# Banded attention: two heads share a transpose of their global columns, P*V runs three units behind, and GpSimd splits the values of pair 1

## The chip, the cores and the metric

The kernel runs on one core of a Trainium2 chip. The metric is the device time of one execution in microseconds (us), median of several. A core has five engines with queues of their own that run in program order and meet only at semaphores: TensorE (PE, with its weight loads PEld), VectorE (DVE), ScalarE (ACT), GpSimd (POOL) and SyncE (SP), which here issues transfers.

## The reference, cut to what matters

Attention with ALiBi biases over a band of 96 local keys and 8 global ones, and two feed-forward layers behind it (a dense one and a mixture of four experts), which the change does not touch.

```python
B, H, S, D = 2, 8, 768, 64
scores = scale * q @ k^T                          # per batch and head
rel = pos[:, None] - pos[None, :]
is_global = pos[None, :] < n_global               # 8
is_local = (rel >= 0) & (rel < n_local)           # 96
dist = where(is_global & ~is_local, n_local, abs(rel))
scores = where(is_global | is_local, scores - slope[h] * dist, -1e9)
a = exp(scores - max); a = a / (sum(a) + 1e-9)
x = (a @ v)                                       # then moe(x), then moe2(x)
```

## The kernel before, in words

**Tiling.** Heads go in pairs: 8 pairs, numbered m = 2i + slot. A pair is 12 units: unit u is query tile u // 2 (128 rows, six of them) of head u % 2. With the band, query tile 0 needs one block of 128 keys, tile 1 two, and tiles 2 to 5 (units 4 to 11) three: two blocks of 128 and the first GLOBAL_COLS = 32 keys. So the scores of such a unit are 288 columns wide.

**One unit's way.** PE multiplies q and k into PSUM (`scores_of_two`, L541, both heads of a tile together). DVE adds the bias and takes the row maximum (`biased`, L1109, instruction at L1117). ACT exponentiates (`expo`, L849). PE transposes blocks of 128 columns (`turn`, L578): one, two or three. The third block is the 32 global columns and 96 columns of zeros that were written once at the start (L1043). ACT copies the transposed blocks to float16 (L890), DVE writes the rest that float16 lost (L1228). PE multiplies with the values (`pv`, L597), three matmuls a block: high by high, high by low, low by high. After six units DVE divides by the sums (`output`, three steps L1149, L1153, L1157).

**Order.** It is written out by hand. In the step of unit u, PE does `turn(u)`, after odd units `scores_of_two` for u + 3 and u + 4, then `pv(u - 2)`, and in steps 0, 2, 4, 6 a transpose of the next pair's q or k (`fill`, L501). DVE does `biased(u + 2)`, the low half of unit u, and what else is due: `output` steps in u = 8, 9, 10 and in u = 1, 2, 3 of the next pair, and a piece of x (`x_low`, L1213) in u = 10 of pairs 4, 5 and 6. ACT does the copy of unit u, `expo(u + 2)`, and its own extras (`values_sum` L873, `weights_sum` L865 in units 21 to 28 and 33 to 40 of the whole count).

**The values.** Each pair's v must be scaled and split into a high and a low float16 part before its `pv`. The scale of pair 0 comes from its own maximum, the scale of all the others from the maximum over all pairs, which is known in step u = 7 of pair 0. Both maxima go over the partitions with a custom GpSimd instruction, `partition_all_reduce` (L790); DVE waits for each of them in its own queue (L1205 for the second) and makes the scale from it. Pair 0 and pair 1 are split by ACT (`values_high`, L857) and DVE (`values_low`, L1187), pairs 2 to 7 by GpSimd (L795 to L802). GpSimd's queue is: index tables by iota, `partition_all_reduce` twice, pairs 2 to 7, then the weights of the dense layer.

Of the kernel before, what the change touches and what calls it, by code (L numbers as in the profile page):

```python
# [13 lines left out]
P = 128  # L14
# [22 lines left out]
def program(nc, q, k, v, n_global, n_local, w_in, w_out, probs, w1, w2, out):  # L37
# [5 lines left out]
    QT = S // P  # L43
# [24 lines left out]
    BAND_COLS = sum(BAND_W[:3])  # L68
    MASK = -8.0e9
# [3 lines left out]
    with ExitStack() as ctx:  # L73
# [93 lines left out]
        kT_sb = [scratch(S) for _ in range(2)]  # L167
        assert at <= hid32.shape[1]
# [7 lines left out]
        W = 3 * P  # L176
        dist_b, key_b = (scratch(BAND_COLS) for _ in range(2))
        s_b = [scratch(W) for _ in range(3)]
        pT_b = [scratch(W).bitcast(F16).rearrange("p (s n) -> p s n", s=2) for _ in range(3)]
# [3 lines left out]
        rel_b = dist_b  # L183
# [52 lines left out]
        v_pairs_max = sem("v_pairs_max")  # L236
        band_ready = sem("band_ready")
# [106 lines left out]
        FILL_AT = [0, 2, 4, 6]  # L344

# [22 lines left out]

        def p_out(u, banded):

            if not banded:
                return bank[2][:, 0:S], pT_g
            n = len(band[u // 2]) * P
            return psum(4 + u % 2, n), pT_b[u % 3][:, :, 0:n]
# [35 lines left out]
        def _(sp):  # L410
# [73 lines left out]
        def _(pe):  # L484
# [27 lines left out]
            def score_parts(i, slot, u, banded):  # L512

                blks = (band if banded else full)[u // 2]
# [16 lines left out]
                head = slice(a * D, (a + 1) * D)  # L531
                return [(psum(u % 3, n, at) if banded else bank[0][:, at:at + n],
# [34 lines left out]
            def turn(i, slot, u, banded):  # L567
# [3 lines left out]
                src = s_b[u % 3] if banded else s_g  # L571
# [5 lines left out]
                for b in range(len((band if banded else full)[u // 2])):  # L577
                    last = pe.transpose(dst[:, b * P:(b + 1) * P], src[:, b * P:(b + 1) * P], ident[:])  # L578
                last.then_inc(pT_psum, 1)

            def pv(i, slot, u, banded):
# [3 lines left out]
                pe.wait_ge(pT_act, UNITS * m + u + 1)  # L585
                pe.wait_ge(pT_dve, UNITS * m + u + 1)
                if u == 0:
                    pe.wait_ge(v_split, m + 1)
                if u in (0, UNITS // 2):
# [3 lines left out]
                keys = [kt for kt, _ in (band if banded else full)[qt]]  # L593
                dst = psum(6 + u // (UNITS // 2), VD, (u % (UNITS // 2)) * VD)
                for b, kt in enumerate(keys):
                    for n, (x, y) in enumerate(((0, 0), (0, 1), (1, 0))):
                        last = pe.matmul(dst, pt[:, x, b * P:(b + 1) * P], v_parts(m)[:, y, a, kt],  # L597
                                         start=(b == 0 and n == 0), stop=(b == len(keys) - 1 and n == 2))
# [22 lines left out]
            def pair(i, slot, banded):  # L621
                for u in range(UNITS):
# [3 lines left out]
                    if banded:  # L626
                        ahead, behind = reach(i, slot, u, 3), reach(i, slot, u, -2)
                        if ahead and u % 2:
                            scores_of_two(*ahead)
                        if not after(i, slot) and u >= UNITS - len(EARLY):  # L630
# [120 lines left out]
        def _(pool):  # L751
# [33 lines left out]

            for n in range(PAIRS):
# [9 lines left out]
                pool.wait_ge(v_part, 3 * n - 5)  # L796
                pool.tensor_scalar(hi, src, 1.0, 1.0, ALU.mult, ALU.mult).then_inc(v_part, 1)
                pool.wait_ge(v_part, 3 * n - 4)
                pool.tensor_tensor(lo, src, hi, ALU.subtract).then_inc(v_part, 1)
                pool.wait_ge(v_part, 3 * n - 3)  # L800
# [30 lines left out]
        def _(act):  # L831
# [13 lines left out]
            def expo(i, slot, u, banded):  # L845
                act.wait_ge(s_ready, PB * i + UNITS * slot + u + 1)
                width = offsets((band if banded else full)[u // 2])[1]
                t = (s_b[u % 3] if banded else s_g)[:, 0:width]
                act.activation(t, t, ACT.Exp, bias=nmax[:, u:u + 1], scale=-1.0).then_inc(p_ready, 1)  # L849

            def values_high(n):

                act.wait_ge(v_scale, n + 1)
                src, hi = v_pieces(n)[0:2]
# [610 lines left out]
```

## Time and profile before

| what | us |
|---|---|
| median of 3 runs (lowest, highest) | 903.66 (902.88, 904.01) |
| the profiled execution, whole | 902.35 |
| its span, first to last instruction | 900.5 |
| PE busy in the span | 873.6 (97%) |
| DVE, ACT, POOL busy | 483.3, 319.2, 257.6 |
| last `pv` of the attention starts | 148.3 |

The profile is of one execution. Times in its views are counted from the first instruction. Of the whole span, attention takes the first 149 us; the two feed-forward layers the rest. [...] The lines in the views are those of the kernel before. "Issue" is time in which an engine waited for nothing that the profile shows.

### The profile page before, as it was taken

Reading aid. Unit: us, or ns where it says so; the run is one execution under the profiler, and the core shown is the slowest. Engines: PE = TensorE matmul, PEld = TensorE weight load, DVE = VectorE, ACT = ScalarE, POOL = GpSimd, SP = SyncE. Lnnn points to the kernel's source line nnn. Section 1 sums busy time; section 2 is a strip of 40 time slices with the busy share of each in tenths; the row PEclk is TensorE's granted clock in tenths of the full one; section 3 lists DMA queues with packets and bytes.
Section 4 is the critical chain, followed back from the end, with each engine's and each line's share of the span. In section 5 each row is a group of like instructions: output and inputs, shape, how many; then the busy total and the mean of one; then the engine's idle time right before and its main releaser. Section 6 shows DMA issues by size and latency. Waiting matters only on the chain.

```text
span 900.5 us, 12637 instructions
## 1 busy us (share of the span) xinstructions
PE 873.6 (97%) x4916; PEld 444.9 (49%) x4916; DVE 483.3 (54%) x1010; ACT 319.2 (35%) x597; POOL 257.6 (29%) x218
## 2 busy tenths in 40 slices
PE   6888999999999999999999999999999999999998
PEld 6666876444444444444444444444444444444443
DVE  7756887999999989874542125222134322212121
ACT  4898886545555656552021110102010111101020
POOL 1278993222222222210029200077000292000000
PEclk9987999999999999999999999999999999999999
DMA  9871420000000000202000500001300000000001
GB/s 214 276 237 37 142 84 1 1 1 1 1 7 3 1 1 1 97 1 94 10 1 0 186 1 1 6 0 53 134 1 6 0 0 0 1 24 23 35 12 49
DMA packets 52004, 39.19 MB, mean 44 GB/s; under 512 B 40816, under 2 KB 41712, under 8 KB 51440
## 3 DMA queue, kind: packets, MB, share of 16 engines
q1 hardware_dynamic: 49888, 34.31, 12.5%
q10 hardware_dynamic: 2064, 4.19, 1.3%
q8 instruction: 31, 0.51, 0.3%
q14 instruction: 21, 0.17, 0.1%
HBM read 35.35 MB, written 3.15 MB: 43 GB/s over the span
## 4 chain that ended last, share of the span: by engine, by line
PE 89%; ACT 5%; DVE 4%; issue 1%; POOL 0%; DVEq 0%
PE bank L607 67%; PE bank L676 14%; PE bank L546 2%; PE bank L578 2%; ACT scaled L865 2%; PE bank L597 2%; ACT tmp L849 1%; ACT tmp L890 1%; PE bank L501 1%; DVE xT L1213 1%; PE bank L559 1%; DVE tmp L1117 1%; ACT hid L839 0%; DVE tmp L1228 0%; DVE tmp L1346 0%
## 5 line engine op out<-in xcount | busy, mean ns | idle before, releaser
L961 ACT ACTIVATE hid<-bank 128x512 f16<-128x512 f32 x96 | 57.3, 597 | 422.2 <-PE bank L607 422.2
L607 PE MATMUL bank<-xT,wA 128*128 128x512 f16 (+1 forms) x864 | 194.6, 379 | 0.0
L1337 DVE SCALAR_TENSOR_TENSOR hid<-bank,hid 128x512 f16<-128x512 f32 x96 | 66.4, 691 | 181.8 <-ACT hid L961 181.8
L607 PEld LDWEIGHTS bank<-xT,wA 128*128 128x128 f16 x864 | 84.5, 98 | 100.6
L676 PE MATMUL bank<-hid,wB 128*128 128x512 f16 x576 | 132.2, 379 | 0.9 <-DVE xT L1213 0.9
L607 PE MATMUL bank<-xT,wB 128*128 x576 | 125.3, 379 | 0.0
L607 PE MATMUL bank<-wA,hid 128*128 128x512 f16 x576 | 125.3, 379 | 0.0
L607 PE MATMUL bank<-wB,hid 128*128 128x512 f16 x576 | 125.3, 379 | 0.0
L815 POOL TENSOR_TENSOR tmp<-tmp 128x512 f32<-128x512 f32 x48 | 61.4, 1280 | 190.2 <-DVE tmp L1360 190.2
L770 POOL TENSOR_SCALAR stage<-stage,sc 128x1024 f32<-128x1024 f32 x32 | 36.0, 1124 | 256.7 <-DVEq L1330 250.4
L1417 DVE SCALAR_TENSOR_TENSOR acc<-bank,pg,acc 128x512 f32<-128x512 f32 x36 | 27.0, 750 | 131.7 <-PE bank L607 131.7
L676 PEld LDWEIGHTS bank<-hid,wB 128*128 128x128 f16 x576 | 56.3, 98 | 69.1 <-DVE xT L1213 1.4
L607 PEld LDWEIGHTS bank<-xT,wB 128*128 128x128 f16 x576 | 56.4, 98 | 67.9
L607 PEld LDWEIGHTS bank<-wA,hid 128*128 128x128 f16 x576 | 56.4, 98 | 68.0
L607 PEld LDWEIGHTS bank<-wB,hid 128*128 128x128 f16 x576 | 56.3, 98 | 68.0
L1228 DVE SCALAR_TENSOR_TENSOR tmp<-bank,tmp 128x384 f16<-128x384 f32 (+2 forms) x96 | 47.0, 490 | 32.7 <-ACT tmp L890 31.6
L607 PE MATMUL bank<-xT,hid 128*128 (+1 forms) x288 | 63.6, 379 | 0.0
L578 PE MATMUL bank<-ident,tmp 128*128 128x128 f32 x240 | 46.8, 296 | 8.1 <-DVE tmp L1228 6.0
L980 ACT ACTIVATE hid<-tmp 128x512 f16<-128x512 f32 x48 | 30.2, 629 | 67.6 <-POOL tmp L815 67.5
L849 ACT ACTIVATE tmp<-tmp 128x288 f32<-128x288 f32 (+2 forms) x96 | 48.5, 506 | 15.6 <-DVE tmp L1117 14.6
L607 PEld LDWEIGHTS bank<-xT,hid 128*128 128x128 f16 x288 | 28.2, 98 | 34.0
L970 ACT ACTIVATE tmp<-bank,sc 128x512 f32<-128x512 f32 x48 | 32.6, 682 | 33.9 <-PE bank L607 30.8
(111 smaller groups left out, 948.8 us busy)
## 6 DMA issues: line engine op xcount, KB each, us to landing
stage<-in_moe_w SPq DMA_DIRECT2D x8, 2048.0 KB, 9.8
stage<-in_moe_w_in SPq DMA_DIRECT2D x1, 4096.0 KB, 16.6
wB<-in_moe_w_out ACTq DMA_DIRECT2D x1, 4096.0 KB, 16.3
hid<-in_q SPq DMA_DIRECT2D x16, 192.0 KB, 3.4
hid<-in_k SPq DMA_DIRECT2D x16, 192.0 KB, 3.5
xT<-in_v SPq DMA_DIRECT2D x8, 384.0 KB, 5.0
out_y<-acc SPq DMA_DIRECT2D x12, 256.0 KB, 2.0
rows<-max SPq DMA_DIRECT2D x4, 128.0 KB, 4.1
```

The source lines that it names most:

```text
L578: last = pe.transpose(dst[:, b * P:(b + 1) * P], src[:, b * P:(b + 1) * P], ident[:])
L607: last = pe.matmul(dst, lhs(c, a), rhs(c, b), start=(c == 0 and n == 0), stop=(c == chunks - 1 and n == 2))
L676: last = pe.matmul(psum(4 + d), w_out_s[:, a, f // 2, f % 2, d * P:(d + 1) * P], hv[:, T % RING, b, :], start=(f == 0 and n == 0), stop=(f ...
L770: pool.tensor_scalar(tmp, src, scale, 1.0, ALU.mult, ALU.mult).then_inc(w_part, 1)
L815: pool.tensor_tensor(g_t[T % 4], g_t[T % 4], r_t[T % 2], ALU.mult).then_inc(g_ready, 1)
L849: act.activation(t, t, ACT.Exp, bias=nmax[:, u:u + 1], scale=-1.0).then_inc(p_ready, 1)
L961: act.activation(hv[:, f, 0, :], psum(f % 4), ACT.Relu).then_inc(f_hi, 1)
L970: act.activation(u_t[T % 2], psum(T % 4), ACT.Exp, scale=inv_h).then_inc(u_ready, 1)
L980: act.activation(hv[:, m % RING, 0, :], g_t[m % 4], ACT.Copy).then_inc(h_hi, 1)
L1228: dve.scalar_tensor_tensor(pt[:, 1], src, P_SCALE, pt[:, 0], ALU.mult, ALU.subtract).then_inc(pT_dve, 1)
L1337: dve.scalar_tensor_tensor(hv[:, f, 1, :], psum(f % 4), 0.0, hv[:, f, 0, :], ALU.max, ALU.subtract).then_inc(f_ready, 1)
L1417: last = dve.scalar_tensor_tensor(y, psum(4 + j), pg[:, j:j + 1], y, ALU.mult, ALU.add)
```

## The change

It touches attention with the band alone, in three ways.

Of units 4 to 11, the odd one of each tile now has its global columns first, so that the 32 global columns of head 0 and those of head 1 lie side by side in one buffer of 576 columns. Each unit transposes its two full blocks; the odd one transposes in addition the 64 shared columns, with the rows of head 0 in partitions 0 to 31 and those of head 1 in 32 to 63. The product with the values uses all 64 rows at once, so a second layout of v is needed (`vg`): v of the first 32 keys of head 0 in partitions 0 to 31, of head 1 in 32 to 63, zeros in the other head's place. It is loaded by two more transfers and split on GpSimd, pair 0 first, the other seven later. Six small steps set it up, and ACT copies a second bias table (288 columns).

`pv` runs three units behind instead of two, with four buffers instead of three, and `output` moves by one step with it.

The values of pair 1 are split by GpSimd, not by ACT and DVE.

```diff
-        s_b = [scratch(W) for _ in range(3)]
-        pT_b = [scratch(W).bitcast(F16).rearrange("p (s n) -> p s n", s=2) for _ in range(3)]
+        s_two = [scratch(2 * W) for _ in range(2)]
+        pT_b = [scratch((2 + n % 2) * P).bitcast(F16).rearrange("p (s n) -> p s n", s=2) for n in range(4)]
...
                 if n == 0:
                     load_pair(0, 1)
+                    for a, rows_a in enumerate((FIRST, SECOND)):
+                        sp.dma_start(vg_all[rows_a], v_d[0:GLOBAL_COLS, a * QT::2 * QT]).then_inc(vg_loaded, 16)
...
+                if banded and far(u):
+                    two = s_two[u // 2 % 2]
+                    start = W + GLOBAL_COLS if u % 2 else 0
+                    for b in range(2):
+                        last = pe.transpose(dst[:, b * P:(b + 1) * P], two[:, start + b * P:start + (b + 1) * P], ident[:])
+                    if u % 2:
+                        last = pe.transpose(dst[0:2 * GLOBAL_COLS, 2 * P:3 * P],
+                                            two[:, W - GLOBAL_COLS:W + GLOBAL_COLS], ident[:])
...
-                        ahead, behind = reach(i, slot, u, 3), reach(i, slot, u, -2)
+                        ahead, behind = reach(i, slot, u, 3), reach(i, slot, u, -PV_LAG)
...
+            def split_second_heads(n, pairs):
+
+                pool.wait_ge(v_scale, n + 1)
+                src = vg_all[:, pairs]
+                pool.tensor_scalar(src, src, scale_cols(v_col(n))[2][BOTH], 1.0, ALU.mult, ALU.mult).then_inc(vg_part, 1)
+                pool.wait_ge(vg_part, 5 * n + 1)
+                for a, rows_a in enumerate((FIRST, SECOND)):
+                    src, hi, lo = vg_all[rows_a, pairs], vg[rows_a, 0, a, pairs, 0:D], vg[rows_a, 1, a, pairs, 0:D]
+                    pool.tensor_scalar(hi, src, 1.0, 1.0, ALU.mult, ALU.mult).then_inc(vg_part, 1)
...
+                    pool.tensor_tensor(lo, src, hi, ALU.subtract).then_inc(vg_part, 1)
...
+            pool.wait_ge(iotas, 3)
+            pool.memset(vg, 0.0).then_inc(vg_ones, 1)
...
+            pool.wait_ge(vg_loaded, 32)
             for n in range(PAIRS):
                 col = v_col(n)
+                if n == 2:
+                    split_second_heads(1, slice(1, PAIRS))
+                if n == 1:
+                    split_second_heads(0, slice(0, 1))
                 if n < 2:
                     pool.wait_ge(v_max, n + 1)
                     pool.partition_all_reduce(scale_cols(col)[0], part[:, 4:5] if n else vpart[:, 0:1], P,
                                               ABSMAX).then_inc(v_amax, 1)
+                if n == 0:
                     continue
+                if n == 1:
+                    pool.wait_ge(v_scale, 2)
                 src, hi, lo, ones, zeros = v_pieces(n)
                 pool.wait_ge(v_split, n)
...
-                    if before(i, slot) is None and u == PAIRS:
-                        values_high(1)
...
-            OUTPUT_AT = UNITS // 2 + 2
+            OUTPUT_AT = UNITS // 2 + PV_LAG
...
-                    if banded and 1 <= u < 4 and before(i, slot):
-                        output(*before(i, slot), 1, u - 1)
+                    at = u - PV_LAG + 1
+                    if banded and 0 <= at < 3 and before(i, slot):
+                        output(*before(i, slot), 1, at)
```

[...] Before:

```order
L762 IOTA tmp 128x32
L790 ISA
L790 ISA sc<-vpart 128x1
L790 ISA sc<-sc 128x1
L795 ISA
L795 TENSOR_SCALAR xT<-xT,sc 128x768
L797 TENSOR_SCALAR xT<-xT 128x12x64
L799 TENSOR_TENSOR xT<-xT 128x12x64
```

After (L867 is `partition_all_reduce`, L842 to L848 `split_second_heads` on `vg`, L875 to L879 the split of a pair, from pair 1 on):

```order
L814 IOTA tmp 128x32
L853 MEMSET hid 64x2080
L856 MEMSET hid 32x8 x2
L867 ISA
L867 ISA sc<-vpart 128x1
L842 ISA
L842 TENSOR_SCALAR hid<-hid,sc 64x64
...
L867 ISA
L867 ISA sc<-sc 128x1
L875 ISA
L875 TENSOR_SCALAR xT<-xT,sc 128x768
```

[...]

The queue of PE in pair 0, steps 6 and 7 (L578 before is `turn`, L546 the scores, L597 `pv`, L501 `fill`). Before:

```order
L578 MATMUL bank<-ident,tmp 128x128 x3
L597 MATMUL bank<-xT,tmp 128x65 x9
L501 MATMUL bank<-ident,hid 128x128 x2
L578 MATMUL bank<-ident,tmp 128x128 x3
L546 MATMUL bank<-hid 128x256 x2
L546 MATMUL bank<-hid 128x32 x2
L597 MATMUL bank<-xT,tmp 128x65 x9
```

After (L612 and L614 are `turn`, L614 the shared one; L578 is now the scores, L645 `pv`):

```order
L612 MATMUL bank<-ident,tmp 128x128 x2
L645 MATMUL bank<-xT,tmp 128x65 x6
L532 MATMUL bank<-ident,hid 128x128 x2
L612 MATMUL bank<-ident,tmp 128x128 x2
L614 MATMUL bank<-ident,tmp 64x128
L578 MATMUL bank<-hid 128x256 x2
L578 MATMUL bank<-hid 128x32 x2
L645 MATMUL bank<-xT,tmp 128x65 x6
L645 MATMUL bank<-hid,tmp 128x65 x3
```

An even and an odd unit have five transposes together instead of six, and as many matmuls with the values as before, which now belong to the unit before.

The queue of DVE in step u = 10 of pair 4 and behind it (L1117 is `biased`, L1228 the low half, L1157 the last step of `output`, L1213 `x_low`). Before:

```order
L1228 SCALAR_TENSOR_TENSOR tmp<-bank,tmp 128x384
L1157 TENSOR_TENSOR acc<-bank,tmp 128x384
L1213 TENSOR_TENSOR xT<-bank,xT 128x512
L1117 ISA tmp<-bank,tmp 128x128
L1117 ISA tmp 128x1
```

After (L1304 the low half, L1231 and L1235 steps of `output`, L1289 `x_low`, L1195 `biased`):

```order
L1304 SCALAR_TENSOR_TENSOR tmp<-bank,tmp 128x256
L1231 RECIPROCAL tmp<-tmp 128x6
L1289 TENSOR_TENSOR xT<-bank,xT 128x512
L1195 ISA tmp<-bank,tmp 128x128
L1195 ISA tmp 128x1
L1304 SCALAR_TENSOR_TENSOR tmp<-bank,tmp 128x384
L1235 TENSOR_TENSOR acc<-bank,tmp 128x384
```

The last step of `output` moved one unit back, behind `x_low` and the next low half.

## Rows read from the trace of the kernel before

**Rows 1.** The page: who holds the chain that ended last; PE's clock in 40 slices

```profile
PE 89%; ACT 5%; DVE 4%; issue 1%; POOL 0%; DVEq 0%
...
PEclk9987999999999999999999999999999999999999
```

**Rows 2.** Stretches of 10 us: busy time, granted clock, DMA share, GB/s

```profile
core 0: us, PE busy (x) PEld busy (x) DVE busy (x) ACT busy (x) POOL busy (x), PEclk, DMA share, GB/s
70.00:80.00 10.00, 9.16 (x58) 7.45 (x60) 4.68 (x20) 10.00 (x24) 9.57 (x8) 0.51 0.01 2
100.00:110.00 10.00, 9.41 (x118) 7.62 (x117) 8.44 (x33) 8.35 (x20) 9.56 (x8) 1.00 0.60 177
180.00:190.00 10.00, 10.00 (x49) 4.52 (x47) 9.26 (x14) 5.42 (x10) 2.54 (x2) 1.00 0.01 2
```

**Rows 3.** The chain that ended last, in time, pair 4: start, us, what

```profile
92.04 0.66 PE bank L501 x4
...
96.12 0.36 PE bank L578 x3
...
97.16 0.33 PE bank L578 x3
...
102.51 0.22 DVE acc L1157
...
102.97 0.68 DVE xT L1213
...
104.47 0.30 PE bank L578
...
106.40 0.66 PE bank L501 x4
```

**Rows 4.** Timeline of POOL to 43 us: start, us, instruction, idle before and releaser

```profile
2.99 0.24 POOL L760 IOTA tmp<- 128x128 f32 x1
...
3.41 0.15 POOL L760 IOTA tmp<- 128x32 f32 x1
...
12.98 0.41 POOL L790 PARTITION_ALL_REDUCE sc<-vpart  x1 [9.32 <-DVE vpart L1251]
27.85 0.36 POOL L790 PARTITION_ALL_REDUCE sc<-sc  x1 [14.46 <-DVE sc L1203]
39.51 0.90 POOL L795 TENSOR_SCALAR xT<-xT,sc 128x768 f32<-128x768 f32 x1 [11.30 <-issue]
...
43.12 0.16 POOL L802 MEMSET xT<- 128x12 f16 x1
```

**Rows 5.** Instructions of L790 and L795: ns min/median/max, first and last start

```profile
L790 POOLq MODIFY_POOL_CONFIG  x2: 6/6/6, 3.6 to 3.6; - x2
...
L795 POOLq MODIFY_POOL_CONFIG  x2: 83/83/83, 28.2 to 28.2; - x2
```

**Rows 6.** Timeline of DVE: what GpSimd waits for, and what waits for it

```profile
11.89 0.95 DVE L1251 TENSOR_REDUCE vpart<-xT 128x1 f32<-128x768 f32 x1
...
28.24 0.15 DVE L1057 TENSOR_SCALAR sc<-sc 128x1 f32<-128x1 f32 x1 [0.49 <-POOL sc L790]
...
33.07 0.07 DVE L1191 MEMSET xT<- 128x12 f16 x1
```

**Rows 7.** Stretches in which POOL changes its library, columns as in the second group

```profile
14.00:25.00 11.00, 8.19 (x76) 6.93 (x75) 8.96 (x25) 8.83 (x21) 0.00 (x0) 0.84 1.09 248
28.20:39.50 11.30, 8.12 (x107) 6.52 (x105) 9.47 (x39) 7.92 (x19) 0.01 (x1) 1.00 1.02 380
4.00:13.00 9.00, 8.08 (x50) 7.32 (x50) 6.06 (x18) 2.50 (x6) 0.02 (x1) 1.00 1.14 258
```

**Rows 8.** The chain that ended last, in time, pair 0 into pair 1

```profile
30.10 0.92 ACT xT L857
...
31.98 0.93 DVE xT L1187
...
38.74 0.20 PE bank L597 x3
```

More of the change, by code:

```diff
@@ L68, in program, with far, unit_blocks, table_at @@
     BAND_COLS = sum(BAND_W[:3])
+    W = BAND_W[2]
+    def far(u):
+        return u // 2 >= 2
+    def unit_blocks(u):
+        blks = band[u // 2]
+        return blks[-1:] + blks[:-1] if far(u) and u % 2 else blks
+    def table_at(u):
+        return BAND_COLS if far(u) and u % 2 else BAND_AT[u // 2]
     MASK = -8.0e9
@@ L367, in reach, with unit_cols, s_b @@
             return other and (*other, (u + ahead) % UNITS)
+        def unit_cols(u, banded):
+            return offsets(unit_blocks(u) if banded else full[u // 2])[1]
+        def s_b(u):
+            at = W * (u % 2)
+            return s_two[u // 2 % 2][:, at:at + unit_cols(u, True)]
         def p_out(u, banded):
@@ L512, in score_parts @@
             def score_parts(i, slot, u, banded):
-                blks = (band if banded else full)[u // 2]
+                blks = unit_blocks(u) if banded else full[u // 2]
                 qt, a = u // 2, u % 2
@@ L531, in score_parts @@
                 head = slice(a * D, (a + 1) * D)
+                runs.sort(key=lambda run: -run[1])
                 return [(psum(u % 3, n, at) if banded else bank[0][:, at:at + n],
@@ L576, in turn @@
                     pe.wait_ge(pT_dve, at - 1)
-                for b in range(len((band if banded else full)[u // 2])):
-                    last = pe.transpose(dst[:, b * P:(b + 1) * P], src[:, b * P:(b + 1) * P], ident[:])
+                if banded and far(u):
[6 more added lines that the diff above has]
+                                            two[:, W - GLOBAL_COLS:W + GLOBAL_COLS], ident[:])
+                else:
+                    src = s_b(u) if banded else s_g
+                    for b in range(len((band if banded else full)[u // 2])):
+                        last = pe.transpose(dst[:, b * P:(b + 1) * P], src[:, b * P:(b + 1) * P], ident[:])
                 last.then_inc(pT_psum, 1)
@@ L584, in pv @@
                 qt, a = u // 2, u % 2
[L585 to L586 removed]
+                shared = banded and far(u)
+                needs = u + 1 - u % 2 if shared else u
+                pe.wait_ge(pT_act, UNITS * m + needs + 1)
+                pe.wait_ge(pT_dve, UNITS * m + needs + 1)
                 if u == 0:
                     pe.wait_ge(v_split, m + 1)
+                if shared and u == 4 and m < 2:
+                    pe.wait_ge(vg_split, m + 1)
                 if u in (0, UNITS // 2):
@@ L626, in pair @@
                     if banded:
-                        ahead, behind = reach(i, slot, u, 3), reach(i, slot, u, -2)
+                        ahead, behind = reach(i, slot, u, 3), reach(i, slot, u, -PV_LAG)
                         if ahead and u % 2:
                             scores_of_two(*ahead)
+                        if not after(i, slot) and u == UNITS - 1:
+                            pv(*behind, banded)
+                            pv(i, slot, UNITS - 3, banded)
+                            behind = None
                         if not after(i, slot) and u >= UNITS - len(EARLY):
```

89 lines of the change are left out of this document (51 added, 38 removed).

## The prediction

> **What bounds the kernel now.** I read three views in this order. First the page: PE holds 89% of the chain that ended last, and its clock is full but for a few slices of the attention [rows 1]. The feed-forward layers are PE without a gap (180 to 190 us: 10.00 of 10 us busy [rows 2]); the change can only move when they start, at 149 us. So what counts is the length of the attention. Second the stretches of the attention: from 100 to 110 us PE is busy 9.41 us, ACT 8.35, DVE 8.44, so PE sets the pace; from 70 to 80 us ACT is busy 10.00 us (it sums weights there) and PE waits at 0.51 of its clock [rows 2]. Third the chain in time. In pair 4 it runs over PE from 92.04 to 106.40, 14.36 us for 12 units, but for one hole: from 102.51 to 104.47 it goes over DVE's `output` and `x_low` and then ACT [rows 3]. In pair 0 it runs over DVE and ACT, the split of pair 1's values among them [rows 8]. GpSimd is on the chain for well under a microsecond. That is what the reader must not take for granted: between 12.98 and 27.85 us its queue holds nothing at all, and now it gets work there.
>
> **Transposes.** Three transposes take 0.33 or 0.36 us of the chain [rows 3], 0.115 us each. Four a pair go, 0.46 us, in pairs where PE sets the pace; where ACT does, its copy is narrower by the same 128 columns, and I take the same. The matmuls with v stay as many. Seven pairs (pair 0 is hidden by what follows): -3.2 us.
>
> **The hole and the lag.** In pairs 4, 5 and 6 the last `output` step stood ahead of `x_low` and now stands behind it and one more unit. The hole is 1.96 us [rows 3]; it can shrink by nothing, if DVE's sum of work is what makes it, or go. The step removed ahead of `x_low` holds the chain from 102.51 to 102.97, 0.46 us, and the lag gives PE one unit more that needs no fresh data. I take 0.6 us each, -1.8 us (0 to -5.9), and -0.5 us for the short waits of `output` for the last `pv` (0 to -1). Together with the transposes -5.5 us, between -3.2 and -10.1.
>
> **Values of pair 1 off ACT and DVE.** The two pieces are on the chain with 0.92 and 0.93 us [rows 8]. They go: -1.9 us, if GpSimd is in time. In time means by PE's `pv` of unit 0 of pair 1, which now stands in step 3, where `pv` of unit 1 was: 38.74 [rows 8]; less 1.9 and 0.2 for transposes: **36.6 us**. PE waits there in order, with the transposes, scores and fills of all later units behind it, and DVE and ACT can run ahead by two units only.
>
> **GpSimd's queue.** [...] In the trace these are two pairs of MODIFY_POOL_CONFIG, at 3.6 and at 28.2 us [rows 5]. The second is followed by 11.30 us in which L795 does not start, for no reason shown [rows 4]; its semaphore was there at 33.14 [rows 6], 6.4 us before it started at 39.51. The first is hidden: between the last iota and 12.98 there are 9.3 us, and `partition_all_reduce` starts 0.14 us after its data [rows 4, 6]. So a change back to the tensor library costs 11.3 us if it begins when the queue reaches it, and 6.4 us at the least; a change to the other costs at most 9.3 us, with no floor. I take the first reading, since a change that begins only at the wait's end would have shown after 12.84 as well. The order has four such rows now, and the third and fourth are not hidden.
>
> The stream of transfers was at 380 GB/s then and is at 248 where the third change falls [rows 7]; so I take 10.5 us for each change to the tensor library, near the measured row, and 9.0 us for each to the other. Walking the queue:
> - the zeroing of `vg`, 2080 columns, at 0.94 ns a column (iota, 0.24 against 0.15 us for 96 columns more [rows 4]) 2.0 us; with two small ones, the queue is at 6.2 us. Change of 9.0: 15.2, against 12.98 before. It also waits for the two new transfers, which are issued near 9.2 us; I expect them within 15.2 and cost them at nothing; without that cover they would cost up to 1 us.
> - `partition_all_reduce`, 0.3; change, 10.5: 26.0. Five small steps for pair 0, 0.28 us each: 27.4. Change, 9.0: **36.4**, the second `partition_all_reduce`, against 27.85 before. DVE waits for it in its own queue [rows 6], ahead of every bias and every low half, so the attention stands still there for some 7 us (it comes to that point about 1 us late by the first item).
> - 0.3; change, 10.5: 47.2. Pair 1 is split in 3.8 us (39.51 to 43.28 [rows 4]): **51.0**, against 36.6 when PE could use it. The loss at this point is 14.4 us and contains both delays before it, since it is one chain of GpSimd.
> - the seven other heads' columns, 448 instead of 768 columns in five steps, at most 4.4 us; PE needs them four units after 51.0, at 1.2 us a unit 4.8 us. Nothing, or a tie. Later pairs take 3.8 us on GpSimd and over 14 on PE: hidden. The weights' split that follows waits for a scale made in pair 2, and moves with it.
>
> The bounds: all at the measured tops (11.3 and 9.2) give 53.0, a loss of 16.4; 8 and 7.5 give 43.0, a loss of 6.4.
>
> **Clock.** While it waits PE does next to nothing. At 70 to 80 us, where PE waited between short bursts, the clock was at the lower level [rows 2]; after these waits some microseconds of pair 1 would run so. I add 1.0 us (0 to 2).
>
> **What costs nothing.** The two copies on ACT fall into its wait for the scale (1.8 us idle). The transfers bring 128 KB into a queue that is full until 27 us, half a microsecond at most, under the wait for GpSimd. The new transposes need both heads' softmax; with `pv` three behind it is there.
>
> [...]
>
> **Sum.** -5.5 + 14.4 + 1.0 = +9.9 us on the profiled execution's 902.35 (span 900.5 and 1.85 around it), that is 912.2. The median of the runs is 1.3 us above that execution: 903.66 + 9.9 = **913.5 us**.
>
> **Rivals.**
> - *A change of library is short.* If each costs the 6.4 us that lay behind the semaphore: 13.3 after the first sum; 19.7; 21.1; 27.5, so the second `partition_all_reduce` is on time at 28; 34.7; values of pair 1 at 38.5. Loss 1.9 us, and -5.5: **900 us**, faster. For it: the 6.4 itself. Against: in that reading something must have begun at the semaphore, and at 12.98 nothing did. It decides where the sum of the three visible changes falls under some 23 us (then the loss is 5.5). Chance 0.10.
> - *Only the first use costs.* Once a library has been there, changes back are free: only the third of the four costs 11.3, the second maximum is on time and pair 1's values come at 33.2. Then -5.5 less nothing: **898 us**. This is also the case where the added rows do nothing on the chip. For it: the change before iota took 0.1 us. Against: nothing shows a return. Chance 0.05.
> - *The gains are larger, the wait shorter.* 8 us and 7.5 us for the changes (loss 6.4) and the holes closed (-7): no change, about **903.5 us**. Chance 0.05.
> - *Forecast*, GpSimd's chain as walked: 905.5 to 918.5. Chance 0.80.
>
> The range of 8 in 10, **905 to 918.5**, leaves out the two fast rivals and little else. A measurement of this kernel can tell 0.2% from no change, 1.8 us. Faster 0.14, same 0.06, slower 0.80.
>
> **What the profile after would show.** Four pairs of MODIFY_POOL_CONFIG, the second `partition_all_reduce` near 36 us instead of 28, DVE idle before L1057's counterpart by 7 us, the next pair's split starting near 47, PE idle ahead of `pv` of pair 1 for some 6 us; after that pairs 4 to 6 at 13.3 us each or so instead of 14.36, with the hole at 102.5 shorter; the attention's end near 159 instead of 149. If the second maximum is on time, the switch is cheap and the sum is wrong by its largest term. If pairs 4 to 6 keep 14.4 us, the transposes were not on the path.

## The result

| | median us | before, same comparison | ratio, 95% interval |
|---|---|---|---|
| changed kernel (6 runs, 915.37 to 922.78) | 917.16 | 903.31 | 1.0168 (1.0134 to 1.0202) |

The change makes the kernel slower by 13.9 us in the medians. The forecast was 913.5 us, 905 to 918.5: the direction and the place are right, the size is 4 us short, and the reasons are only half right. The runs of the changed kernel spread over 7 us, where those of the kernel before spread over 1.5. The profiled execution is the slowest of them, 922.78 us; its differences are therefore larger than the median's.

The page of the changed kernel, parts 2 and 4 (compare [rows 1]; the feed-forward layers are the same, so is the 89%):

```profile
PEclk9796699999999999999999999999999999999999
...
PE 89%; ACT 4%; DVE 3%; issue 2%; SPq 1%; POOL 0%; DMA 0%; POOLq 0%; DVEq 0%
```

The clock row shows 7, 9, 6, 6 in slices 2 to 5, which reach from 23 to 115 us. The level goes between two values in the traces of both kernels: over stretches of 1 us it is 1.00 or 0.50 of full speed, but for those in which it changes. In the profiled execution the last matmul with the values starts at 169.3 us instead of 149.0, 20.3 us later. How the delay grows is seen at the start of `biased` for unit 6 of a pair: it is 7.6 us late in pair 1, 9.8 in pair 3 (87.6 instead of 77.8 us) and 16.4 in pair 4 (110.6 instead of 94.2). So 6.6 us come between pairs 3 and 4, where the clock is low nearly all the time, and 3.9 us behind that, where it is full. Where the time went is seen in three places.

**First, GpSimd's queue.** Its timeline, and the rows of MODIFY_POOL_CONFIG at L867 (L867 is `partition_all_reduce`, L842 the heads' columns, L875 to L882 the split of pair 1):

```profile
3.72 1.82 POOL L853 MEMSET hid<- 64x2080 f16 x1
...
13.43 0.41 POOL L867 PARTITION_ALL_REDUCE sc<-vpart  x1 [7.52 <-DMA hid<-in_v]
22.58 0.31 POOL L842 TENSOR_SCALAR hid<-hid,sc 64x64 f32<-64x64 f32 x1 [8.74 <-issue]
...
30.77 0.41 POOL L867 PARTITION_ALL_REDUCE sc<-sc  x1 [6.48 <-issue]
41.80 0.90 POOL L875 TENSOR_SCALAR xT<-xT,sc 128x768 f32<-128x768 f32 x1 [10.61 <-issue]
...
45.39 0.16 POOL L882 MEMSET xT<- 128x12 f16 x1
```

```profile
L867 POOLq MODIFY_POOL_CONFIG  x4: 2/6/16, 5.8 to 24.7; - x4
```

These rows come in pairs: L867 has two pairs, L842 one at 13.8 us and L875 one at 31.1. From the last iota to the splits that makes four pairs where the kernel before has two [rows 5], one for each ISA row without operands in the order. I call a switch such a pair together with the time up to the next start: 7.52 us at most, then 8.74, 6.48 and 10.61. The prediction and the expectations say change of library for it; no trace shows what GpSimd does in that time. The second maximum comes at 30.77 us instead of 27.85 [rows 4], pair 1's values at 45.5. DVE stood still for it, and PE behind DVE:

```profile
31.22 0.15 DVE L1133 TENSOR_SCALAR sc<-sc 128x1 f32<-128x1 f32 x1 [3.04 <-POOL sc L867]
```

```profile
32.74 0.80 PE L578 MATMUL bank<-hid 64*128 64x128 f32 x4 [3.97 <-DVE tmp L1195]
```

**Second, the clock.** Stretches of the changed kernel, columns as in [rows 2]:

```profile
30.00:45.00 15.00, 12.26 (x89) 9.04 (x89) 7.21 (x32) 5.52 (x14) 3.44 (x4) 0.59 0.76 284
65.00:85.00 20.00, 18.78 (x145) 13.95 (x145) 10.12 (x42) 16.07 (x39) 12.82 (x17) 0.57 0.21 47
95.00:110.00 15.00, 15.00 (x103) 10.88 (x103) 7.40 (x32) 6.56 (x17) 14.50 (x10) 0.50 0.14 33
112.00:127.00 15.00, 14.46 (x172) 11.45 (x172) 11.17 (x44) 11.61 (x30) 14.21 (x11) 1.00 0.72 217
```

From 95 to 110 us PE is busy without a gap at the lower level, 0.50: 103 matmuls in 15 us, against 172 at the higher one from 112 to 127. In the kernel before, the level was low in the profiled execution from 53 to 60 and from 70 to 80 us, where ACT had no idle time, and for 3.4 us from 19 us on, as in the changed kernel.

**Third, pairs at full clock.** They did not get shorter. DVE's last `output` step of the second half ends a pair; here two of them, of pairs 4 and 5:

```profile
127.00 0.55 DVE L1235 TENSOR_TENSOR acc<-bank,tmp 128x384 f32<-128x384 f32 x1
...
142.01 0.55 DVE L1235 TENSOR_TENSOR acc<-bank,tmp 128x384 f32<-128x384 f32 x1
```

15.01 us a pair, against 14.36 [rows 3]; the forecast said 13.3. One unit of PE in it shows why (L645 is `pv`, 128 rows and then 64; L619 and L532 follow):

```profile
135.30 0.36 PE L645 MATMUL bank<-xT,tmp 128*128 128x65 f16 x6
135.59 0.26 PE L645 MATMUL bank<-hid,tmp 64*128 64x65 f16 x3
135.78 0.33 PE L619 MATMUL bank<-ident,tmp 128*128 128x128 f32 x1
```

And one tile, an even unit and an odd one, in the kernel before, in its timeline of PE (L597 is `pv`, L578 `turn`, L546 the scores):

```profile
114.79 0.45 PE L597 MATMUL bank<-xT,tmp 128*128 128x65 f16 x9
115.08 0.52 PE L578 MATMUL bank<-ident,tmp 128*128 128x128 f32 x3
115.44 0.44 PE L597 MATMUL bank<-xT,tmp 128*128 128x65 f16 x9
115.71 0.53 PE L578 MATMUL bank<-ident,tmp 128*128 128x128 f32 x3
116.17 0.70 PE L546 MATMUL bank<-hid 64*128 64x256 f32 x4
```

From start to start nine products took 0.29 us and now take 0.48. The rows one by one show where: between products over 128 rows a start follows the last by 0.03 us; from the last one over 128 rows to the first over 64 it is 0.125 us, and from the last over 64 to the next transpose 0.12. So each change between 128 and 64 rows costs about 0.1 us, and a unit has two of them more.

The transposes did become cheaper on PE. In the tile above they take 0.36 and 0.46 us, 0.82 together. In the changed kernel they take 0.28 us for two (51.71 to 51.99) and 0.48 for three (52.46 to 52.94), 0.76 a tile:

```profile
51.71 0.44 PE L612 MATMUL bank<-ident,tmp 128*128 128x128 f32 x2
51.99 0.35 PE L645 MATMUL bank<-xT,tmp 128*128 128x65 f16 x6
52.27 0.26 PE L645 MATMUL bank<-hid,tmp 64*128 64x65 f16 x3
52.46 0.44 PE L612 MATMUL bank<-ident,tmp 128*128 128x128 f32 x2
52.73 0.27 PE L614 MATMUL bank<-ident,tmp 128*64 128x128 f32 x1
52.94 0.38 PE L578 MATMUL bank<-hid 64*128 64x128 f32 x2
```

One transpose is 0.11 us; here 0.06 is left of the saving, since the first transpose behind a product over 64 rows takes 0.165 us to the next start instead of 0.141. The shape of the shared transpose, 128*64, costs nothing: its 0.20 us to the start of the scores are the same in the kernel before, with 128*128. But the saving of a tile is small against the 0.4 us of its four changes of rows.

**The chain of pair 5** shows what became of the hole at `x_low` (L619 is `turn`, L1235 the last step of `output`, L532 `fill`):

```profile
139.78 0.23 PE bank L619 x2
...
142.01 0.55 DVE acc L1235
...
143.92 0.44 PE bank L532 x2
```

From 128.91 to 140.01 us it stays on PE, so `x_low` no longer makes a hole. A new one stands at the last step of `output`: for 3.9 us, from 140.01 on, the chain goes over ACT's copies, `expo` and DVE.

### The profile page after: what moved, and what is told of

Same layout as the page of the kernel before. It is cut to its first block, busy times and chain, and to the rows that moved or that the text cites. A ratio compares the mean times of both kernels' runs of the same rounds, so it can differ in the third digit from the quotient of the medians.

```text
span 921.0 us, 12595 instructions
## 1 busy us (share of the span) xinstructions
PE 893.8 (97%) x4884; PEld 453.8 (49%) x4884; DVE 479.4 (52%) x1004; ACT 315.3 (34%) x598; POOL 268.2 (29%) x236
## 4 chain that ended last, share of the span: by engine, by line
PE 89%; ACT 4%; DVE 3%; issue 2%; SPq 1%; POOL 0%; DMA 0%; POOLq 0%; DVEq 0%
PE bank L655 66%; PE bank L728 14%; PE bank L645 3%; PE bank L578 2%; PE bank L612 1%; ACT scaled L942 1%; PE bank L532 1%; ACT tmp L928 1%; ACT tmp L971 1%; PE bank L619 1%; SPq L447 1%; DVE xT L1289 1%; ACT hid L919 0%; DMA hid<-in_v 0%; DVE acc L1235 0%
## 5 line engine op out<-in xcount | busy, mean ns | idle before, releaser
L895 POOL TENSOR_TENSOR tmp<-tmp 128x512 f32<-128x512 f32 x48 | 61.5, 1280 | 200.4 <-DVE tmp L1437 200.4
L1304 DVE SCALAR_TENSOR_TENSOR tmp<-bank,tmp 128x256 f16<-128x256 f32 (+1 forms) x96 | 42.8, 446 | 50.6 <-ACT tmp L971 50.1
L578 PE MATMUL bank<-hid 64*128 64x256 f32 (+2 forms) x320 | 43.4, 387 | 6.5 <-DVE tmp L1195 6.1
L971 ACT ACTIVATE tmp<-bank 128x256 f16<-128x256 f32 (+1 forms) x96 | 38.2, 398 | 32.1 <-PE bank L619 12.4
L655 PEld LDWEIGHTS bank<-xT,hid 128*128 128x128 f16 x288 | 28.2, 98 | 34.0
## 6 DMA issues: line engine op xcount, KB each, us to landing
stage<-in_moe_w SPq DMA_DIRECT2D x8, 2048.0 KB, 10.6
stage<-in_moe_w_in SPq DMA_DIRECT2D x1, 4096.0 KB, 13.3
```

The source lines that it names most:

```text
L578: last = pe.matmul(*parts[a][n], start=True, stop=True)
L655: last = pe.matmul(dst, lhs(c, a), rhs(c, b), start=(c == 0 and n == 0), stop=(c == chunks - 1 and n == 2))
L895: pool.tensor_tensor(g_t[T % 4], g_t[T % 4], r_t[T % 2], ALU.mult).then_inc(g_ready, 1)
L971: act.activation(pt[:, 0], src, ACT.Copy, scale=P_SCALE).then_inc(pT_act, 1)
L1304: dve.scalar_tensor_tensor(pt[:, 1], src, P_SCALE, pt[:, 0], ALU.mult, ALU.subtract).then_inc(pT_dve, 1)
```

## The experiments

Three theories: **L**, GpSimd's switches; **T**, the change of array shape between 128 and 64 rows; **O**, the new lag and the new place of `output`. Beside them the clock, as a cost of its own or as what the others set off. All medians below stand against the kernel before in the same comparison, 904.1 to 904.6 us.

### The whole, less one suspect

**No switch added.** The head columns of pair 0 go to DVE, pair 1 back to ACT and DVE:

```diff
-                if n == 1:
-                    split_second_heads(0, slice(0, 1))
...
-                if n == 0:
+                if n < 2:
                     continue
...
+                if u == 2 and VG_ON_DVE:
+                    heads_of_pair_0()
```

> The changed kernel, but no tensor operation stands on GpSimd ahead of the second all-reduce: the 32 global rows of pair 0 are split by DVE in step 2 of pair 0 (four small instructions), pair 1's values by ACT and DVE as in the kernel before. So two of the four changes of library go. Theory L (the GpSimd chain is the largest loss): the second all-reduce comes back to about 28 us, the first pair's end from 48.4 to about 40, and the median falls by 8 to 12 us against the changed kernel, to 905 to 909; the low-clock stretches at 33 to 46 us go as well. Rival T (the products over 64 rows cost PE the time in every pair): less than 4 us come back, pairs 4 to 6 stay at 15.0 us each under both.

Measured: 915.52 us, ratio 1.0121 (1.0105 to 1.0138), 11.3 us over the kernel before. The second maximum came at 28.41 us, as L said; the first pair ended at 46.8 instead of 48.4 us, and pairs 4 to 6 took 15.0 us. About 2.6 us came back, the rival's amount; since 13.9 and 11.3 us have intervals of about 3 and 1.5 us either way, that is not clear of zero. But the stretch from 30 to 45 us was at the lower level all the same:

```profile
30.00:45.00 15.00, 13.02 (x101) 9.76 (x102) 7.79 (x33) 7.51 (x18) 5.24 (x7) 0.61 0.83 293
```

So with GpSimd's delay gone, slow PE was the next limit at the same place. That alone doesn't say that L is small.

**128 rows for the shared product.** The value layout is zero in rows 64 to 127; the transpose takes 128 columns:

```diff
-                        last = pe.transpose(dst[0:2 * GLOBAL_COLS, 2 * P:3 * P],
-                                            two[:, W - GLOBAL_COLS:W + GLOBAL_COLS], ident[:])
+                        last = pe.transpose(dst[:, 2 * P:3 * P],
+                                            two[:, W - GLOBAL_COLS:W - GLOBAL_COLS + P], ident[:])
...
-                    parts.append((pT_b[(u + 1 - a) % 4][BOTH, :, 2 * P:3 * P], vg[:, :, a, m]))
+                    parts.append((pT_b[(u + 1 - a) % 4][:, :, 2 * P:3 * P], vg[:, :, a, m]))
```

> The changed kernel, but the shared product uses all 128 rows of the array (rows 64 to 127 of the value layout are zero, and the transpose takes 128 columns, of which the last 64 are other finite data), so that PE never changes between 128-row and 64-row matmuls for it. Theory T (each change of array shape costs about 0.1 us, two a unit in pv and one or two a tile in the transposes): pairs 4 to 6 fall from 15.0 to 13.3 to 13.8 us each, the median by 7 to 11 us. Rival L: pairs keep 15.0 us and the median stays within 2 us of the changed kernel's 917.

Measured: 909.9 us, ratio 1.0054 (1.0037 to 1.0071): 5.6 us over the kernel before, so 8 us came back. Pairs 4 to 6 took 14.1 us:

```profile
119.52 0.55 DVE L1235 TENSOR_TENSOR acc<-bank,tmp 128x384 f32<-128x384 f32 x1
...
133.62 0.55 DVE L1235 TENSOR_TENSOR acc<-bank,tmp 128x384 f32<-128x384 f32 x1
```

```profile
122.89 0.36 PE L645 MATMUL bank<-xT,tmp 128*128 128x65 f16 x6
123.09 0.26 PE L645 MATMUL bank<-hid,tmp 128*128 128x65 f16 x3
123.18 0.42 PE L612 MATMUL bank<-ident,tmp 128*128 128x128 f32 x2
```

The nine products take 0.29 us here, from start to start, at the same full clock. The shared transpose now has the shape 128*128 and still takes 0.20 us to the start of the scores:

```profile
126.17 0.27 PE L614 MATMUL bank<-ident,tmp 128*128 128x128 f32 x1
126.37 0.70 PE L578 MATMUL bank<-hid 64*128 64x256 f32 x4
```

The transposes of this tile take 0.25 us (125.31 to 125.56) and 0.44 (125.93 to 126.37), 0.69 against 0.82 in the kernel before: the whole saving of one transpose. T holds for the median, and for the pairs too (0.9 us each), though they end above the 13.3 to 13.8 expected.

**Both edits.**

> Both edits together. If L and T are both true and add up: 893 to 899 us, that is faster than the kernel before by 5 to 10 us, what the prediction counted as the gain of the transposes, the hole and the lag (5.5 us). If the lag or the new place of output costs something of its own, it stays at 900 or above with pairs 4 to 6 above 14 us.

Measured: 904.1 us, ratio 0.9998 (0.9989 to 1.0008). All 14 us come back, and not one of the 5.5 us that the prediction counted as the gain. Removed one by one the two give 2.6 and 8.3 us, together 14.1: 3 us belong to both, since a delay by GpSimd and a slow PE lie beside each other in pair 0 and pair 1. L with T mended is 909.9 - 904.1 = 5.8 us, and 2.6 with T in place. T with L mended is 915.5 - 904.1 = 11.4 us, and 8.3 with L in place. The 5.8 and the 11.4 are differences within one comparison and clear of the noise.

### One suspect alone, in the kernel before

**64 rows for the third block.**

```diff
-                        last = pe.matmul(dst, pt[:, x, b * P:(b + 1) * P], v_parts(m)[:, y, a, kt],
+                        r = slice(0, 2 * GLOBAL_COLS if banded and b == 2 else P)
+                        last = pe.matmul(dst, pt[r, x, b * P:(b + 1) * P], v_parts(m)[r, y, a, kt],
```

> The kernel before with one edit: the product of the third block (global columns) in units 4 to 11 runs over 64 rows instead of 128; the rest is the same. Theory T: each of 64 units pays for two changes of shape, 0.09 to 0.1 us each, 1.5 us in a pair where PE sets the pace, so pairs 4 to 6 take 15.5 to 16 us instead of 14.36, and the median rises by 6 to 11 us. If the shape does not matter: 903, within 1 us.

Measured: 918.9 us (911.2 to 922.8), ratio 1.0172 (1.0126 to 1.0218). This one line, which gives the array fewer rows to use, costs as much as the whole change. A pair takes 15.13 us instead of 14.36:

```profile
113.70 0.55 DVE L1158 TENSOR_TENSOR acc<-bank,tmp 128x384 f32<-128x384 f32 x1
...
128.83 0.55 DVE L1158 TENSOR_TENSOR acc<-bank,tmp 128x384 f32<-128x384 f32 x1
```

0.77 us in eight pairs is 6.2 us; the expectation had 1.5 us a pair, too much, as part of it falls into PE's waits. The rest of the 14.6 us goes with the clock: its four executions took 911.2, 915.05, 922.75 and 922.82 us at mean granted clocks of 0.984, 0.979, 0.972 and 0.972. From the first to the last the time at the lower level grows by 22 us (0.012 of 921 us, halved level, so times two) and the execution by 11.6: half a microsecond for each. At the same mean clock of 0.984 the kernel before took 903.7 to 905.0 us. So the one line costs some 7 us there, and more as the clock falls with it.

**The lag alone.** `pv` three units behind, `output` a step later, four buffers:

```diff
-            OUTPUT_AT = UNITS // 2 + 2
+            OUTPUT_AT = UNITS // 2 + PV_LAG
...
-                    if banded and 1 <= u < 4 and before(i, slot):
-                        output(*before(i, slot), 1, u - 1)
+                    at = u - PV_LAG + 1
+                    if banded and 0 <= at < 3 and before(i, slot):
+                        output(*before(i, slot), 1, at)
```

> The kernel before with one edit: pv three units behind, four buffers for the transposed blocks, and output one step later, as in the changed kernel. The prediction's theory (the hole in pairs 4 to 6 shrinks by about 0.6 us): pairs 4 to 6 fall from 14.36 to 13.8 us and the median by 1 to 2 us. Rival (output's last step in u = 4 falls on the path of the units behind it, as the changed kernel's chain suggests): the hole only moves, pairs 4 to 6 take 14.2 to 14.7 us, the median stays within 1 us.

Measured: 907.5 us, ratio 1.0030 (1.0018 to 1.0042), 2.9 us slower; 14.82 us a pair, worse than both expected. Its chain in time, at the start of a pair (L895 ACT's copy, L854 `expo`, L847 and L844 copies of k and q, L1162 the last `output` step, L1122 the bias):

```profile
112.27 0.47 ACT hid L847
112.74 0.49 ACT tmp L895
...
113.73 0.55 DVE acc L1162
114.27 0.11 DVE tmp L1122
...
114.69 0.54 ACT tmp L854
115.22 0.37 ACT hid L844
...
115.63 0.44 PE bank L502 x2
```

Four microseconds in which the chain never touches PE. The last step of `output` now falls in u = 4, where ACT and DVE have the copies of the next pair's operands too; PE's next transposes wait for them. The hole at `x_low` did not close here either: the chain is off PE from 104.18 to 108.90 us. That hole and this one, from 111.38 to 115.63, are 9 us of a pair of 14.8.

**Two switches alone.** One operation on a single column between the two all-reduces:

```diff
+                if n == 1:
+                    pool.tensor_scalar(bf[:, 6:7], two, 1.0, 1.0, ALU.mult, ALU.mult).then_inc(extra, 1)
+                    pool.wait_ge(extra, 1)
```

> The kernel before with one tiny tensor operation (one column) on GpSimd between the two all-reduces, so that it changes its library twice more, and nothing else. The chain 13.4 + 8.7 + 0.3 + 6.5, from the changed kernel's trace, puts the second all-reduce at 29.2 us instead of 27.9, 1.3 us of wait for DVE: median higher by 1 to 3 us if only the wait counts, by 4 or more if the wait also lets PE's clock fall. If the prediction's 10.5 and 9.0 us were right, the second all-reduce would come at 33.5 us and the median would rise by 5.5 us or more.

Measured: 905.56 us, ratio 1.0009 (1.0000 to 1.0019), about 1 us slower. GpSimd's timeline:

```profile
21.98 0.19 POOL L790 TENSOR_SCALAR bf<-sc 128x1 f32<-128x1 f32 x1 [8.61 <-issue]
28.39 0.41 POOL L794 PARTITION_ALL_REDUCE sc<-sc  x1 [6.22 <-DVE sc L1207]
42.13 0.90 POOL L799 TENSOR_SCALAR xT<-xT,sc 128x768 f32<-128x768 f32 x1 [13.34 <-issue]
```

The one operation brings two more pairs of MODIFY_POOL_CONFIG, at 13.3 and at 22.4 us. 8.6 us for the switch to the tensor operation; the one back was hidden, within 6.2 us, as the second maximum now waited for DVE. By the prediction's 10.5 and 9.0 us it would have come at 33.5. The switch behind it took 13.3 us, the longest of all.

**Pair 1 on GpSimd alone.**

```diff
-                    continue
+                if n == 0:
+                    continue
+                if n == 1:
+                    pool.wait_ge(v_scale, 2)
...
-                    if before(i, slot) is None and u == PAIRS:
-                        values_high(1)
```

> The kernel before with one edit: pair 1's values are split by GpSimd. No library change is added, but the one that is there (11.3 us) is no longer hidden: the values come at 39.5 + 3.8 = 43.3 us and pv of pair 1 needs them at 36.9 less the 1.9 us that ACT and DVE save. Loss 6 to 8 us at that point, so the median rises by 5 to 9 us; if there is slack behind it, less than 3.

Measured: 910.93 us, ratio 1.0066 (1.0049 to 1.0082), 6.4 us slower, within the expected 5 to 9. The switch that was hidden in the kernel before is on the path here, where pair 1 depends on it: L798 started 10 us behind the all-reduce, at 37.94, and the values were there at 41.7.

### The clock, and the fastest version

**Filling the wait of pair 0.** In the changed kernel, 14 matmuls of the identity in step 7 of pair 0:

> The changed kernel with 14 matmuls of the identity (3 to 4 us, unused) in step 7 of pair 0, where PE waits 4 us for the second all-reduce. Clock theory: the level stays high from 32.7 to 46.3 us, pair 0 ends 4 to 6 us earlier and the median falls by 3 to 6 us. Rival (the level falls anyway, by the shape of the work): no change or up to 1 us slower.

```diff
+                    if banded and (i, slot, u) == (0, 0, 7):
+                        pe.wait_ge(tr_out, 2 * FILLS)
+                        hold(psum(3, P), 14)
```

Measured: 914.95 us, ratio 1.0132 (1.0115 to 1.0150), against 917.16. The low level ended at 33.7 instead of 46.3 us, but pair 0 ended at 47.9 and not at 42 to 44: PE, fast now, came to pair 1's values early and waited for GpSimd. (Each of the 14 stands as two rows in the trace.)

```profile
28.96 5.02 PE L596 MATMUL bank<-ident 128*128 128x128 f32 x28 [2.72 <-ACT hid L930]
33.91 0.84 PE L578 MATMUL bank<-hid 64*128 64x256 f32 x8
...
45.92 0.25 PE L650 MATMUL bank<-xT,tmp 128*128 128x65 f16 x3 [1.28 <-POOL xT L890]
```

The added matmuls also held the scores up by 1.2 us (33.91 against 32.74). The clock did as expected and the time did not: in pair 0 two limits of the same length lie beside each other, and removing one shows almost nothing. In the profiled execution the low stretch of 17 us from 94 to 111 is missing too; with four runs here and a spread of 7 us in the changed kernel, the 2 us between the medians are not certain.

**The old place of `output`.** On the kernel with both edits:

```diff
-                    at = u - PV_LAG + 1
-                    if banded and 0 <= at < 3 and before(i, slot):
-                        output(*before(i, slot), 1, at)
+                    for at in {2: (0, 1), 3: (2,)}.get(u, ()):
+                        if banded and before(i, slot):
+                            output(*before(i, slot), 1, at)
```

> The third kernel (no library changes added, product over 128 rows) with output of the second half back to its old place in time: its first two steps both in u = 2 and the last in u = 3 of the next pair, instead of u = 2, 3, 4. Theory O (the last step in u = 4 holds the bias of unit 6 and the copy of the next pair's q behind it, which is what made the lag alone cost 0.46 us a pair): pairs 4 to 6 fall from 14.11 to 13.5 us or less, the median from 904.1 to 899 to 901. Rival (the chain over ACT's copies sets the pace whatever DVE does): 14.0 or more a pair, no change of the median.

Measured: 903.47 us, ratio 0.9998 (0.9987 to 1.0009); 14.02 us a pair instead of 14.11. Theory O falls in this form: putting the step back a unit gives 0.1 us, so where that one step stands is not what holds the pair; that it is the chain over ACT's copies, `expo` and DVE as a whole is what its views suggest, not shown. Why the lag alone costs 0.46 us a pair is left open beyond that; its chain shows where, not which of its parts.

**Keeping PE busy where ACT sets the pace**, three more matmuls of the identity a unit, in that kernel and in the kernel before:

```diff
+                    if at in range(22, 30) or at in range(34, 42):
+                        hold(dst[:, 0:P], 3)
```

> The same, and in units 22 to 29 and 34 to 41, where ACT sums the weights and PE waits, PE does three more matmuls of the identity a unit before it waits for its transposes; nothing uses them. Clock theory (the low level that the trace shows at 60 to 84 us comes from PE waiting there, and lasts into stretches where PE is needed): no low level between 55 and 90 us, pairs 2 and 3 shorter by 1 to 4 us, median 896 to 899. Rival: the added matmuls stand in the way (0.3 us a unit), no gain or a loss of up to 3 us.

> The kernel before with the same three matmuls of the identity in units 22 to 29 and 34 to 41. In it the low level stands at 53 to 60 and 70 to 80 us, nearly all of it where ACT sets the pace, so by the clock theory little is to be had: 0 to -2 us, and the low level goes from these stretches. If the matmuls cost time themselves: +1 to +4 us.

Measured: 902.32 us, ratio 0.9983 (0.9974 to 0.9991), and 904.66 us, ratio 1.0007 (0.9997 to 1.0016). The low level went from 55 to 90 us in both. Pairs 2 and 3 are as long as without (19.5 and 15.9 us), so there the level cost nothing in the profiled executions. Against the same kernel without the added matmuls the spread is smaller (901.5 to 903.1 us against 901.7 to 905.1) and the median 1.2 us lower; the 896 to 899 expected is not reached. For the kernel before nothing; the low level there lay where ACT sets the pace.

**And in units 6 to 11 of pair 0**, four more a unit:

```diff
+                    if at in range(6, 12):
+                        hold(dst[:, 0:P], 4)
```

> The kernel with three added matmuls of the identity a unit in the weight-summing stretch, and four more a unit in units 6 to 11 of pair 0, where PE waits for the second maximum, its scale and pair 1's values, and where the level is low from 31.9 to 38.7 us in the profile of the kernel without them. Clock theory: the level stays high from 25 us on, pair 0 and 1 end 2 to 3 us earlier, median 899 to 901. Rival: PE is needed in these units and the added matmuls (0.9 us a unit at the high level) stand in its way: level high, but no gain or a loss of up to 3 us.

Measured: 901.3 us, ratio 0.9968 (0.9956 to 0.9979), 2.8 us under the kernel before: the best version, just above the 899 to 901 expected. Its stretches show the high level where the kernel with both edits had 0.77 and 0.74:

```profile
30.00:45.00 15.00, 14.44 (x187) 12.33 (x185) 11.51 (x46) 11.93 (x30) 5.13 (x7) 1.00 0.79 287
65.00:85.00 20.00, 18.79 (x233) 16.66 (x230) 12.28 (x49) 19.20 (x45) 17.73 (x15) 1.00 0.21 47
```

Pair 0 ends at 39.9 us instead of 42.3 in the one before it, and everything behind moves with it. Here, with GpSimd out of the way, the clock theory holds for pair 0; of the median the four matmuls a unit give 1.0 us. They were not added to the kernel before, which has a low stretch of 6.8 us in pair 0 as well (32 to 39 us in the run with three more a unit). So it is not shown that the 2.8 us belong to the change; they may be the clock's alone.

## Why the prediction was right or wrong

**GpSimd's chain** (14.4 us in the sum): the mechanism was right, the four rows of the order were four switches on the chip, and the second maximum and pair 1's values came late in this order. The term was mis-sized. The switches to tensor operations took 8.7 and 10.6 us where it had 10.5, the one back 6.5 where it had 9.0, which no run shows: I had taken a ceiling (9.3 us, with no floor) as the value. The values of pair 1 came at 45.5 us and PE took them at 46.5, so 9.9 us late against 36.6. Of the median this is 2.6 us (not clear of the noise) if the rest of the change stays, and 5.8 us if the array shape is mended first. The expected idle time of PE of some 6 us ahead of that `pv` did not show: PE at the lower level came no earlier.

**The transfers and the zeroing** cost less than said: the first all-reduce at 13.43, 0.45 us late, held by the transfer of `vg`; the switch before it was over within 7.5 us.

**The transposes** (-3.2 us): right on PE in its mechanism, 0.06 us a tile as the change stands and 0.13 with all products over 128 rows, for the 0.115 forecast. But the pairs did not become shorter by it: with both edits, a pair at full clock is 0.25 us shorter than before, where transposes, hole and lag were to give 1.1. No run removes the transposes alone, so their share of the median is not shown.

**"The matmuls with v stay as many"** was the step that failed. Their number did, their price did not: three over 64 rows between others over 128 made nine cost 0.48 instead of 0.29 us. I costed it at nothing and gave no bound, though the order had it in plain sight (`hid`, the 64-row value layout, as operand of every third product). By the runs it is the largest single part, 8.3 us, or 11.4 with GpSimd mended, the clock that comes with it included. The traces show about 0.1 us at each change of rows (0.19 us for the two around the shared products); for a change from 128 to 64 columns they show no price, 0.20 us to the start of the scores behind either.

**The hole and the lag** (-2.3 us): wrong in sign. The hole at `x_low` is off the chain in the changed kernel, where PE has more to do, but it is there with the lag alone (4.7 us) and with both edits (115.52 to 119.96 us); and another opened at `output` in all three. The lag alone costs 2.9 us. Its bounds, "0 to -5.9", left out a loss for no reason. Putting `output` back gave 0.1 us a pair, so what makes the loss stays open.

**The clock** (+1.0 us): right that it belongs in the sum, far too small. In the profiled execution the lower level held 48 us of the attention, 14 + 17 + 17, beside 3.4 us near 20 us; in the kernel before 17 us, 7 + 10, beside the same 3.4. In the runs the mean granted clock is 0.970 to 0.981, against 0.984 to 0.990. With 0.976 and 0.988 as middle values that is an estimated 22 us more at the lower level, and at half a microsecond each, as far as PE sets the pace, up to 11 of the 13.9 us. This is no part beside the others: it is how the wait for GpSimd and the shape reach the median, and no run of the changed kernel holds the clock up throughout, which would tell the two apart. The prediction also read the row from 70 to 80 us as a wait, where PE is busy 9.16 of 10 us, slowly; the gaps lay ahead of it, with 1.19 of 2.20 us busy from 68.0 on. The changed kernel's slowest two runs, 922.5 and 922.8 us, are also those with the lowest clock. What sets the level off is not settled beyond this: it went where the added matmuls stood, and it was low behind waits of a few microseconds or work with gaps (in the changed kernel PE was busy 0.52 of 4.70 us from 28.0 on, 2.01 of 3.60 from 63.0, 2.82 of 4.30 from 90.0; in the kernel before 1.87 of 3.00 from 50.0).

**The rivals.** A short switch was given 0.10. The measured ones (8.7, 6.5, 10.6) lie between its 6.4 and the forecast's 10.5, but for the last. The reading that counts from the semaphore (6.4 us) falls: in the changed kernel the second maximum waited with its data there, and L842 had its scale from about 14.7 us, 7.9 us ahead of its start. The rival's 6.4 us is near the switch to the all-reduce, 6.5 (6.2 to 7.5 where one was seen), and not met by those to tensor operations, 7.5 to 13.3 in the traces here.

In the medians, with the shape mended first, the account is: GpSimd 5.8 us where the forecast had 14.4, the gains nothing where it had 5.5, the shape 8 where it had nothing, and the clock inside these where it had 1.0. That is 8.6 too much, 5.5 and 8 too little, 1 too much: the errors cancelled to 4 us. That the forecast lay near the result is luck in that sense; only its sign rests on a mechanism that the runs bore out in kind.

## What to carry to other kernels

- A matmul over 64 rows of the array was not cheaper here between neighbours over 128 (nine products in 0.48 us against 0.29): padding it to their 128 rows with zeros saved 8 us. Look at the shape column of the trace beside the count.
- Ahead of an edit that puts work on GpSimd, look for ISA rows without operands in the order and for MODIFY_POOL_CONFIG in the trace, and ask of each whether anything waits behind it; two kinds of operation in turn cost 6 to 13 us a turn here, and a switch that was hidden is not free once a consumer depends on what follows: with pair 1 behind it the median rose by 6.4 us.
- Where two limits lie beside each other (a late engine and a slow clock), remove both before either is judged; and where PE's clock falls in a wait, matmuls that nobody uses can be worth more than they take (2.2 us here, from 903.47 to 901.3, with everything else mended).

## What the runs showed of the hardware

- A change between 128-row and 64-row matmuls costs about 0.1 us each way at full clock (starts 0.125 and 0.12 us apart instead of 0.03). A 128*64 fp32 transpose among 128*128 ones costs nothing extra: 0.11 us ahead of it and 0.20 us to the scores behind it, as with 128*128.
- GpSimd's switch to tensor operations took 7.5 to 13.3 us in 14 traces, with no clear tie to the rate of the transfers: 7.5 at 286 GB/s, 8.7 at 248, 10.0 at 371, 11.3 at 380, 13.3 at 321. The switch to the all-reduce took 6.2, 6.5 and 7.5 us where it was not hidden. It did not wait for the data of the next instruction: in the changed kernel the queue came to the second one at 24.3 us, the data of the all-reduce were there at 28.2, and it started at 30.8, 6.5 us behind the first and 2.6 behind the second.
- The lower level of TensorE's clock came in stretches of 3.4 to 24 us; in one and the same kernel the mean level ran from 0.972 to 0.984, and the time with it over 11.6 us.
